# A fourth double place for attention's scores, and the last weights read in 8 KB pieces with one pair of sums for all experts

## What is computed

```python
# attention, per head (q pooled over 2 rows by their mean)
scores = scale * q_pool @ k.T
attn = exp(scores - max(scores)); attn /= sum(attn) + 1e-9
x = attn @ v                                   # 2304 x 512 in all
# first mixture
P = exp(x @ w_gate - max); 8 rounds of row and column normalisation
for e in range(8): out += P[:, e:e+1] * (relu(x @ w1[e]) @ w2[e])
# second mixture, on out as its x
d = exp(x @ phi - max over rows); d /= sum over rows
slot_input = d.T @ x                           # 32 slots x 512
for e in range(8): slot_out[e] = relu(slot_input[e] @ s_w1[e]) @ s_w2[e]
c = exp(x @ phi - max over slots); c /= sum over slots
result = c @ slot_out
```

## Time and profile before

| what | value |
|---|---|
| median of 3 runs | 1806.49 us (1805.34 to 1807.61) |
| the profiled execution | 1804.97 us |
| its span, first to last instruction | 1803.2 us |
| TensorE busy | 1745.8 us (97%) |
| VectorE busy | 1000.2 us (55%) |
| ScalarE busy | 778.2 us (43%) |
| GpSimd busy | 428.8 us (24%), nearly all in attention |
| mean granted TensorE clock | 0.983 |

### The profile page before, as it was taken

How to read it: one execution, slowest core, us unless ns; L and a number is a source line. 1 busy time by engine, 2 the same in 40 slices (tenths; PEclk the granted TensorE clock), 3 DMA queues, 4 the chain that set the end, 5 groups by cost and what they waited for, 6 DMA issues and landing times.

```text
span 1803.2 us, 32013 instructions
## 1 busy us (share of the span) xinstructions
PE 1745.8 (97%) x13337; PEld 1309.6 (73%) x13337; DVE 1000.2 (55%) x1291; ACT 778.2 (43%) x1163; POOL 428.8 (24%) x326
## 2 busy tenths in 40 slices
PE   7999999999999999999999999999999999999885
PEld 6777777777766787777777777777777777777354
DVE  6766667666654455555555555555555555555211
ACT  3444444444446544444444444444444444444101
POOL 3778877787760000000000000000000000000000
PEclk9999999999999999999999999999999999999976
DMA  9532131231007344444443443444434444545998
GB/s 275 157 73 47 41 80 41 63 58 41 28 2 269 131 150 152 138 139 136 139 150 129 152 141 136 139 140 137 150 129 152 140 138 140 184 163 195 368 387 308
DMA packets 178815, 258.59 MB, mean 143 GB/s; under 512 B 46704, under 2 KB 65136, under 8 KB 178032
## 3 DMA queue, kind: packets, MB, share of 16 engines
q1 hardware_dynamic: 178672, 256.54, 44.0%
HBM read 251.79 MB, written 9.96 MB: 145 GB/s over the span
## 4 chain that ended last, share of the span: by engine, by line
PE 60%; DMA 4%; ACT 2%; DVE 2%; SPq 1%; issue 1%; DVEq 0%
PE ring L997 42%; PE ring L1007 6%; PE ring L1019 4%; PE pv L1054 3%; DMA wring<-in_moe_w_dram 2%; DVE w_lo L1293 1%; ACT w_hi L1186 1%; PE ring L909 1%; SPq L882 1%; PE ring L920 1%; DMA hring<-in_moe_w_dram 1%; DMA xraw<-in_moe_w_dram 1%; PE ring L1105 1%; DMA out_dram<-wring 1%; PE ring L1054 1%
## 5 line engine op out<-in xcount | busy, mean ns | idle before, releaser
L997 PE MATMUL ring<-w_hi,x_split 128*128 128x512 f32 x2304 | 790.9, 404 | 3.3 <-DVE w_lo L1293 2.5
L997 PEld LDWEIGHTS ring<-w_hi,x_split 128*128 128x128 f32 x2304 | 432.9, 188 | 116.6 <-issue 24.6
L997 PE MATMUL ring<-w_lo,x_split 128*128 128x512 f32 x1152 | 450.0, 391 | 0.0
L1293 DVE TENSOR_TENSOR w_lo<-w_raw,w_hi 128x1024 fp32r<-128x1024 f32 x288 | 356.7, 1239 | 154.9 <-ACT w_hi L1186 154.9
L1231 ACT ACTIVATE wring<-ring,pw 128x512 f32<-128x512 f32 x218 | 149.9, 688 | 436.0 <-PE ring L997 436.0
L1335 DVE COPY h_t<-ring 128x512 f32<-128x512 f32 x288 | 199.2, 692 | 237.0 <-PE ring L1007 236.9
L552 POOL TENSOR_TENSOR acc<-acc,pt 128x576 f32<-128x576 f32 x217 | 307.2, 1416 | 31.1 <-ACT pt L413 1.8
L1186 ACT ACTIVATE w_hi<-w_raw 128x1024 fp32r<-128x1024 f32 x288 | 302.2, 1049 | 0.0
L485 DVE TENSOR_REDUCE neg_part<-ring 116x2 f32<-116x768 f32 (+1 forms) x240 | 228.3, 958 | 90.5 <-PE ring L293 81.5
L1474 POOL TENSOR_TENSOR x_split<-xraw,x_split 128x512 fp32r<-128x512 f32 (+1 forms) x20 | 23.5, 1180 | 980.5 <-ACT x_split L1178 980.5
L997 PEld LDWEIGHTS ring<-w_lo,x_split 128*128 128x128 f32 x1152 | 217.5, 189 | 37.8
(11 more groups left out here) (218 smaller groups left out, 1736.6 us busy)
## 6 DMA issues: line engine op xcount, KB each, us to landing
w_raw<-in_moe_w_dram SPq DMA_DIRECT2D x288, 512.0 KB, 3.5
wring<-in_moe_w_dram SPq DMA_DIRECT2D x37, 1024.0 KB, 11.8
xraw<-in_moe_w_dram SPq DMA_DIRECT2D x10, 1024.0 KB, 14.3
q_raw<-in_q_dram SPq DMA_DIRECT2D x32, 288.0 KB, 5.6
v_raw<-in_v_dram SPq DMA_DIRECT2D x16, 576.0 KB, 4.5
k_raw<-in_k_dram SPq DMA_DIRECT2D x30, 288.0 KB, 7.2
hring<-in_moe_w_dram SPq DMA_DIRECT2D x6, 1024.0 KB, 14.5
spare<-in_moe_w_dram SPq DMA_DIRECT2D x5, 1024.0 KB, 16.3
```

The lines of the kernel that those rows point to most:

```text
L997: last = pe.matmul(h_ps[n % 3][:, :], a[:, k, toks], w[:, k, :], start=(k == 0 and m == 0), stop=(k == DK - 1 and m == 2))
L1293: dve.tensor_tensor(w1_lo[v % 2][:, 2 * c:2 * c + 2, :], w1_raw[:, 2 * (p % RAWS):2 * (p % RAWS) + 2, :], w1_hi[v % 2][:, 2 * c:2 * c + 2, ...
```

## The change

In attention the banks of `pv` and `misc` become the two halves of a fourth double place, `ring[3]`. While the row phase runs, every fourth item (positions 2, 6, 10 and so on, but none of the last three) goes to it; all others go round the three old places. Every item of the row phase but the first and the last few thus takes a place that was used four items before. Position 2 waits besides until ScalarE has copied the product with v (`o_kept`) and VectorE has read the sums of the half before the last (`guarded`). After the row phase TensorE waits until the last item in the fourth place has been read. `add_keys` stands behind the first two steps of `times_v` instead of ahead of them. A pair's nat items are given to its halves as 9 and 6.

At the end, all 48 loads and the spare copies read 8 KB for each partition that lie together, and write 8 KB that lie together; products and transposes take each fourth column in turn where the order of rows changed so. The last load comes in two parts of 4 KB for each partition. The output store puts 2 rows of 2 KB together. The slots' first products of all experts are summed in two banks: the slots of the other experts are zero in `si_own`, each load is used by 4 products (2 pieces of the inner dimension x 2 banks) that keep to two groups of 32 columns, and there is one evacuation and one turning for each bank at the end in place of one for each expert. The last block's `product` uses three banks in turn.

```diff
-    BUFS = 3
+    BUFS = 4
-    NAT_HALF = [0, 8, NATS]
+    NAT_HALF = [0, 9, NATS]
...
-    NUMBER = {x: n for n, x in enumerate(IN_RING)}
+    FOURTH = {x for n in range(LAST_HALF + 1) for i, x in enumerate(row_phase(n)) if i % BUFS == 2 and i < len(row_phase(n)) - 3}
+    LAST_FOURTH = [[x for x in row_phase(n) if x in FOURTH][-1] for n in range(LAST_HALF + 1)]
+    PLACE, WAS = {}, {}
+    for x in IN_RING:
+        PLACE[x] = BUFS - 1 if x in FOURTH else sum(1 for y in PLACE if y not in FOURTH) % (BUFS - 1)
+        WAS[x] = [y for y in WAS if PLACE[y] == PLACE[x]][-1:]
...
+        pv, misc = ring[3][:, 0, :], ring[3][:, 1, :]
...
-                for kind, a, i in row_phase(n):
+                for at, (kind, a, i) in enumerate(row_phase(n)):
+                    if at == 2 and n >= 1:
+                        pe.wait_ge(o_kept, n)
+                    if at == 2 and n >= 2:
+                        pe.wait_ge(guarded, n - 1)
                     put(kind, a, i)
+                read(*LAST_FOURTH[n])
...
-                if n >= 1:
-                    add_keys(n - 1)
                 for j in range(KT):
                     times_v(n // 2, KT * (n % 2) + j)
+                    if j == 1 and n >= 1:
+                        add_keys(n - 1)
...
-    s_w1_u = s_w1.rearrange("e (k p) (n f) -> e n p k f", p=P, n=2)
-    s_w2_u = s_w2.rearrange("e (n j p) d -> e n p j d", p=P, n=2)
+    w2_rows = w2.rearrange("e (u p j) d -> e u p j d", p=P, u=HALVES)
+    s_w1_rows = s_w1.rearrange("e (p n k) (u f) -> e n p k u f", p=P, n=2, u=HALVES)
+    s_w2_rows = s_w2.rearrange("e (n p j) d -> e n p j d", p=P, n=2)
...
-                sp.dma_start(place, rows).then_inc(arrived, 16)
+                if k == LOADS - 1:
+                    sp.dma_start(place[:, 0:FB // 2, :], rows[:, 0:FB // 2, :]).then_inc(arrived, 16)
+                    sp.dma_start(place[:, FB // 2:FB, :], rows[:, FB // 2:FB, :]).then_inc(last_in, 16)
+                else:
+                    sp.dma_start(place, rows).then_inc(arrived, 16)
...
-                product(NB - 1, q, h_ps[q % 2])
+                if q >= 3:
+                    pe.wait_ge(g_added, QUADS * (NB - 1) + q - 2)
+                product(NB - 1, q, h_ps[q % 3])
...
-                    for k in range(DK):
-                        last = pe.matmul(h_ps[n][k * SLOTS:(k + 1) * SLOTS, :], si_t[:, k, :], weights[:, k, :], start=True, stop=True)
-                    last.then_inc(part_made, 1)
+            def first_product(e, n):
+                weights, arrived, count = tail(first_load(e, n))
+                pe.wait_ge(arrived, count)
+                for k in (2 * n, 2 * n + 1):
+                    for u in range(2):
+                        last = pe.matmul(h_ps[u][k * SLOTS:(k + 1) * SLOTS, :], si_own[:, e, k, :], weights[:, 2 * (k % 2) + u, :],
+                                         start=(e == 0), stop=(e == E - 1))
+                last.then_inc(part_made, 1)
...
-            for e in range(E):
-                first_product(e)
-                if e >= 1:
-                    turn_parts(e - 1)
-            turn_parts(E - 1)
+            for e in range(E):
+                for n in range(2):
+                    first_product(e, n)
+            for u in range(2):
+                turn_parts(u)
+            pe.wait_ge(h2_kept, 2)
```

More of the change, by code:

```diff
@@ L222, in _, with read @@
         def _(pe):
-            def place(kind, p, n):
-                at = NUMBER[kind, p, n]
-                if at >= BUFS:
-                    was, a, m = IN_RING[at - BUFS]
-                    if was == "s":
-                        pe.wait_ge(exp_done, STEPS * a + m + 1)
-                    elif was == "nat":
-                        pe.wait_ge(max_done, NAT_NUMBER[a, m] + 1)
-                    else:
-                        pe.wait_ge(low, TURN_NUMBER[a, m] + 1)
+            def read(kind, p, n):
+                if kind == "s":
+                    pe.wait_ge(exp_done, STEPS * p + n + 1)
+                elif kind == "nat":
+                    pe.wait_ge(max_done, NAT_NUMBER[p, n] + 1)
+                else:
+                    pe.wait_ge(low, TURN_NUMBER[p, n] + 1)
+            def place(kind, p, n):
+                for last in WAS[kind, p, n]:
+                    read(*last)
                 return buffer(kind, p, n)
@@ L786, in split_place @@
             return t.bitcast(F32)
-        PLACES = [("x", rows_of_x(i), TT) for i in range(3)] \
+        PLACES = [("x", behind_c(i), TT) for i in range(3)] \
             + [("slots", four(i), last_user(i)) for i in EARLY_RING] \
```

113 lines of the change are left out of this document (50 added, 63 removed).

## The result

The changed kernel takes 1761.1 us (median), the kernel before, run beside it, 1805.9 us. Three of its four runs took 1759.83 to 1761.15 us; the fourth took 9541.12 us and is left out of the ratio. The ratio is 0.9748, with a 95% interval of 0.9729 to 0.9767. The forecast was 1762 us, and the profiled execution took 1759.83 us (span 1758.0) against 1760.6 in the prediction's sum.

The account below looks back on a forecast made before the run. Attention was taken as bound by TensorE stalling on three places for VectorE's maximum, the end by transfers. Attention -35.0 and end -9.4 make -44.4 from 1804.97, 1760.6; runs' median stands 1.5 higher, so 1762 us, range 1752 to 1775.

Parts of the forecast that it names:

- row phases of 14 pairs: Attention, halves 2 to 29: with four places items run unstalled, 2.3 us less per pair, -32.2 us.
- half 1: Attention: 11 nat and 9 s items take 13.29 us against 10.7 unstalled; -1.7 of the 2.6 us taken.
- half 0: Attention, no row in the trace: gain between 0 and -2.6 us, taken as -0.5.
- first nat item waits for the split: Attention, a pair's second half: later `add_keys` delays VectorE's split, 0.1 us for each of 14, +1.4, range 0 to +5.6.
- `add_keys` in halves 29 to 31: Near attention's end: two steps of `times_v` cover its 0.67 us wait for ScalarE's copy of the maxima, three times, -2.0 us.
- loads: The end: 8 KB pieces move at 419 in place of 386 GB/s, 37 loads x 0.214 = -7.9 us.
- last load in two parts: The end: only half a step is left behind the last landing, -1.0 us.
- stores: The end: 4 KB pieces for the output stores, about -0.5 us, from 0 to -1.
- Rival 1: The end: slots' first products fall behind at clock 0.5, costing about 7 us, up to 20; about 1769 us; chance 0.12.
- Rival 2: The end: larger pieces bring nothing, the end is worth -1.5, time 1770 us; chance 0.07.
- Rival 3: Attention: stalls move instead of going, half of the 35 us stays, 1780 us; chance 0.11 (0.01 of it at 1797).
- Rival 4: Attention: GpSimd becomes the bound and the kernel slower; at 0.5 us more per addition 1843 us; chance 0.02.

Follow-up runs that it names:

- end_small: Changed kernel with three small end edits undone (last load in one part, store rows of 2 KB apart, product over two banks); 1761.2 us.
- short_max: Kernel before, three places, with each maximum reading 2 x 192 in place of 2 x 384 numbers; 1776.4 us, ratio 0.9837.
- nat_8: Changed kernel with a pair's nat items given to its halves as 8 and 7, as before; 1770.6 us, ratio to before 0.9804.
- nine_stages: Changed kernel with one place for each of the nine stores in place of four; 1760.5 us, ratio to before 0.9752.
- attn_only: Kernel before with only the attention part of the change; 1769.85 us, ratio 0.9802.
- pool_plus1: Changed kernel with one addition more for each half on GpSimd; 1768.6 us, ratio to before 0.9793.
- pool_plus2: Changed kernel with two additions more for each half on GpSimd; 1811.5 us in one run.
- pieces_2k: Changed kernel with loads and spare copies in the row order of before, 2 KB pieces; 1769.0 us, ratio to before 0.9799.
- no_fourth: Changed kernel with all row-phase items on three places, no fourth place; 1786.0 us, ratio to before 0.9891.
- end_only: Kernel before with only the end's part of the change; 1794.8 us, ratio 0.9939.

## Why the prediction was right, step by step

| step | predicted, us | measured in the traces, us |
|---|---|---|
| row phases of 14 pairs | -32.2 | 14 x (20.11 - 17.85) = -31.6 |
| half 1 | -1.7 | 13.29 to 12.28: -1.0 |
| before half 0 | 0 | +0.3 |
| half 0 | -0.5 | 13.47 to 12.76: -0.7, but +1.3 by the clock behind it |
| first nat item waits for the split | +1.4 | 0 |
| `add_keys` in halves 29 to 31 | -2.0 | -2.3 |
| rest of the second halves | 0 | 13 x 0.11 = -1.4 |
| last `add_keys` waits for VectorE | 0 | +1.1 |
| attention | -35.0 | -34.4 |
| loads | -7.9 | 104.5 to 95.7: -8.8 |
| last load in two parts | -1.0 | 3.1 (`end_small`) to 2.7: -0.4 |
| clock behind the last landing | 0 | 4.5 to 3.1: -1.4 |
| stores | -0.5 | -0.4 |
| the end | -9.4 | -11.0 |

**The sum.** 1760.6 us against 1759.83 in the trace is closer than the terms are. Six rows are off by 0.9 to 1.4 us, in both directions, and cancel. That part is luck; that the row phases and the loads make up 40 of the 45 us, for the reasons given, is not.

**The row phases.** The mechanism is as told: three places against 0.73 + 0.97 us. The distances between items were 0.53, the 112 waits went, and `short_max` reached nearly the same by VectorE's time. But the step was right for a reason that it did not contain. It called the phases unstalled with four places, whatever the split of the nat items. `nat_8` shows that with the old split the place would have brought 1.6 us of the 2.36 per pair: one item of each phase would still have taken its place from a maximum three items back, which the step did not look at, and the small operations would have stood between two maxima. "Unstalled" held for 9 and 6 only. Had the change left the split at 8 and 7, the same argument would have been 9.5 us too good. That the split was right as well is luck, as far as the prediction goes.

**The wait for the split.** The step took 0.1 us for each of 14 and allowed up to 0.4. The 14 waits are there, 6.5 us in sum, and cost nothing: in the changed kernel the split ends at 363.89 + 0.28 = 364.17 us (two rows of VectorE below), and the nat item that needs it starts at 364.22. That is just in time: the last 28 matmuls of `times_v` and the start of the next phase are 3.52 us apart in a second half (330.55 to 334.07) and 3.49 in a first half, where nobody waits for the split.

```profile
363.27 0.69 DVE L469 SCALAR_TENSOR_TENSOR q_lo<-ring,q_hi 128x576 fp32r<-128x576 f32 x1
363.89 0.28 DVE L471 TENSOR_TENSOR k_lo<-ring,k_hi 128x128 fp32r<-128x128 f32 x1
```

The bound of 0.3 us was too high: it used L455's 1.16 us for two operations that take 0.90 together from start to end.

**Half 0 and half 1.** Two small losses, both outside the steady pairs that I had rows for. Half 1 keeps a stall of 1.06 us, where VectorE's small operations stand between maxima as in `nat_8`, and one of them (L509) takes 1.31 us beside GpSimd in place of 0.17. Behind half 0's row phase the granted clock fell. The lower clock stands in the window from 36 to 40 us, where the kernel before has 1.00:

```profile
36.00:40.00 4.00, 3.63 (x18) 2.72 (x20) 2.14 (x3) 0.68 (x2) 3.66 (x3) 0.59 1.00 370
```

**The last `add_keys`.** The prediction asked who waits for VectorE behind a later `add_keys` within the steady pairs, and not at the end of the loop, where the next `add_keys` follows at once and VectorE adds beside GpSimd. That is a missed term, 1.1 us, and two other terms of the same edit (1.4 and 0.3 more than booked) hid it. The 1.4 stands in the second halves, where a few matmuls of queries and keys are too little to cover ScalarE's copy of the maxima; the prediction saw that wait only near the end.

**The loads.** Loads arrived 2.706 us apart before (seven steps between 1761.83 and 1780.77 us) and 2.488 after (eight between 1718.00 and 1737.90 us). For 37 loads that is 8.1 us of the 8.8 measured; the row of the spare units (419 GB/s) was the right one to take the new rate from. The page DMA: Bandwidth & Descriptors of the Trainium skill (Bandwidth) lets the memory's share of 358 GB/s bind; by it the pieces would have brought nothing. The trace disagrees: 387, 410 and 419 GB/s with pieces of 2, 4 and 8 KB are all above that figure, with one core at work. The 425 GB/s that the same page measures, and that the prediction named, are nearer.

**The last load.** Mis-sized, and hidden by the clock. The edit is worth 0.4 us (`end_small`) and not 1.0; half of the 1.98 us step was taken at the lower clock of the row, while the half step at full clock takes 0.69 us and the whole one 1.12. The other 1.4 us are TensorE's clock behind the last landing: 0.50 in the trace of before, 1.00 in that of the changed kernel. The change does not decide it. In `short_max`, whose end is that of before, the step ran at 1.00 and took 1.12 us; in `nine_stages`, with the load in two parts, it ran at 0.50 and took 1.94 us for the whole. So this is luck, and no term had it.

**The rivals.** Rival 1 did not come: the first products ran at a granted clock of 1.00 from 1680 to 1700 us, and `attn_only` shows that a TensorE late by the old form's amount costs nothing there. Rival 2 is out by the pieces' runs. Rival 3, with a margin of 0.40 us too small to hide a wait, is out by the 0.53 us distances. Rival 4's sum was right, and `pool_plus1` and `pool_plus2` give its price: the changed kernel lies 2.3 us per pair away from it. Two small slips of the prediction change nothing: its chances add up to 0.97 faster and 0.02 slower, not 0.96 and 0.03, and the good ends that it names sum to -52.8 us, not -54.

## What to carry to other kernels

Count the time from an item's start to the free place against the distance at which the place is wanted again, and do it for every item of the phase, the last ones too, not for the alternation in its middle alone. Look also at what else stands in the reader's queue between two reads. Here one leftover item for each half and one group of small operations for each pair cost 0.75 us together, nearly half of what the fourth place brought, and the split of work between phases decided both. Where an order is changed in a loop, price the last round by itself, since its neighbours are others. A rate to expect from larger pieces may already stand in the trace of before, in a transfer that happens to have them.

## What the runs showed of the hardware

- **A transfer pays for each piece.** 512, 256 and 128 pieces for 1 MB took 2.71, 2.56 and 2.50 us, 0.0005 to 0.0006 us for each piece, with all DMA engines busy (a share of 1.01 to 1.05). Whether the number of pieces counts or their distance in memory is open.
- **Behind a short idle stretch TensorE's clock was halved, though not always.** In half 0's row phase TensorE stands still once, waiting for a maximum. In the eight kernels with a fourth place in which this lasted 1.80 to 1.83 us, the granted clock fell from 2.4 to 1.2 GHz within 3 us and for some 3 to 4 us in seven, and stayed in one (`pieces_2k`). In the kernel before, `no_fourth`, `end_only` and `short_max` it stood still for 1.68 to 1.78 us in the same place, in `pool_plus1` and `pool_plus2` for 0.23 and 1.45, and the clock stayed in all six. The fall cost 1.3 to 1.6 us. That the same stretch of 1.82 us had both outcomes says that its length alone does not decide; what else does was not tried, and no run tests that the stretch is the cause.
- **Two operands in SBUF make VectorE wait for GpSimd.** In half 0 of the changed kernel L509, a difference of two SBUF operands of 128 x 4 numbers that takes 0.17 us in the steady pairs, took 1.76 us and ended at 34.58 us; GpSimd's addition had begun at 32.70 and ended at 34.55. This made most of the idle stretch of 1.82 us: in `pool_plus1` the same operation (L510, third row below) began 0.01 us ahead of a GpSimd addition and took 0.17 us, and TensorE stood still for 0.23. In `pool_plus2` it began 0.06 us behind one, took 1.39 us and ended with it, and TensorE stood still for 1.45. The form with 128 x 6 numbers takes 1.3 us in nearly every pair of the changed kernel, behind the last maximum of a half. VectorE's maxima, which read PSUM, keep 0.96 us whatever GpSimd does.

```profile
32.82 1.76 DVE L509 TENSOR_TENSOR neg_col<-neg_max,neg_col 128x4 fp32r<-128x4 f32 x1
```

```profile
32.70 1.85 POOL L551 TENSOR_TENSOR q_sum<-q_raw 96x768 f32<-96x768 f32 x1
```

```profile
33.89 0.17 DVE L510 TENSOR_TENSOR neg_col<-neg_max,neg_col 128x4 fp32r<-128x4 f32 x1
```

The Trainium skill (SBUF — State Buffer, "SBUF: two separate sides") describes a port pair that these two engines lock for a whole instruction, also for a VectorE operation with two SBUF inputs; the trace agrees with it here.
